# Attention with a matrix state and two MLP blocks on one core: queries transposed ahead of the kernel and loaded by DMA, in place of transposes on TensorE

## What is computed

```python
# q, k, v: (4, 8, 768, 48), beta: (4, 8, 768), all float32
k_n = k / (norm(k) + 1e-06)
for t in range(768):
    y[:, :, t] = q_t @ state                       # the queries read the state
    v_old = k_t @ state
    state = state + beta_t * outer(k_t, v_t - v_old)
# x = y, heads side by side: (4, 768, 384)
# block 1: mixing along the sequence (x^T U V), then relu(u @ w_ch1) @ w_ch2, both with residuals
# block 2: real part of a 2D FFT, layer norm, then the same kind of MLP
```

## Time and profile before

| | us |
|---|---|
| median of 3 runs | 1266.56 |
| lowest and highest run | 1260.3, 1274.25 |
| span of the profiled execution | 1268.3 |
| TensorE busy in it | 1173.2 |
| VectorE busy | 590.1 |
| ScalarE busy | 449.0 |
| GpSimd busy | 116.1 |

### The profile page before, as it was taken

The page is one execution under the profiler, slowest core; times in us unless marked ns, Lnnn a source line. Parts: engine busy times, 40 slices in busy tenths (PEclk is TensorE's granted clock), DMA queues, the critical chain, the costliest instruction groups (busy, mean ns, idle before and its releaser), DMA issues. The chain is left out here.

```text
span 1268.3 us, 24886 instructions
## 1 busy us (share of the span) xinstructions
PE 1173.2 (93%) x9978; PEld 1118.7 (88%) x9978; DVE 590.1 (47%) x1116; ACT 449.0 (35%) x853; POOL 116.1 (9%) x117
## 2 busy tenths in 40 slices
PE   4699999998999999599999999996799999999998
PEld 3598888888889888499999999995799999999998
DVE  7557776567764673352222222324553433434322
ACT  2566666565665653141211111212231221221211
POOL 4112211122111210000000000000000000000000
PEclk9899999999998997699999999998899999999999
DMA  5111112212112110441010100001111001001001
GB/s 98 26 32 34 31 26 37 39 26 39 22 33 39 51 62 29 127 151 52 1 38 1 37 0 0 1 1 52 48 52 38 19 1 38 19 0 37 19 16 40
DMA packets 98535, 44.87 MB, mean 35 GB/s; under 512 B 78037, under 2 KB 97162, under 8 KB 98314
## 3 DMA queue, kind: packets, MB, share of 16 engines
q1 hardware_dynamic: 98442, 43.47, 13.4%
HBM read 34.03 MB, written 11.85 MB: 36 GB/s over the span
## 5 line engine op out<-in xcount | busy, mean ns | idle before, releaser
L1220 DVE SCALAR_TENSOR_TENSOR hid_l_mix<-up_mix,hid_h_mix 128x384 fp32r<-128x384 f32 x96 | 53.4, 557 | 209.2 <-ACT hid_h_mix L1165 209.2
L382 DVE CAST_PREDICATED zi<-merge_mask,zb 128x512 f16<-128x512 uint8 x144 | 100.5, 699 | 98.8 <-PE zb L630 97.9
L1220 DVE SCALAR_TENSOR_TENSOR hid_l_dft<-up_dft,hid_h_dft 128x384 fp32r<-128x384 f32 x96 | 53.5, 557 | 183.9 <-ACT hid_h_dft L1165 183.8
L1165 ACT ACTIVATE hid_h_dft<-up_dft 128x384 fp32r<-128x384 f32 x96 | 47.2, 492 | 255.8 <-PE up_dft L1330 255.8
L1165 ACT ACTIVATE hid_h_mix<-up_mix 128x384 fp32r<-128x384 f32 x96 | 47.2, 492 | 245.7 <-PE up_mix L1330 245.7
L525 ACT CAST xi<-xb 128x512 f16<-128x512 f32 x144 | 82.3, 590 | 110.5 <-PE xb L656 68.8
L733 PE MATMUL pb<-kq_t,kz 128*128 128x256 f32 x384 | 99.2, 404 | 4.3 <-DVE nr L423 4.2
L1328 PE MATMUL dn_mix<-w2h_mix,hid_h_mix 128*128 128x384 f32 x288 | 99.5, 346 | 3.0 <-DVE hid_l_mix L1220 2.5
L1328 PE MATMUL dn_dft<-w2h_dft,hid_h_dft 128*128 128x384 f32 x288 | 98.5, 342 | 0.1
L1328 PE MATMUL up_mix<-act_h_mix,w1h_mix 128*128 128x384 f32 x288 | 97.1, 337 | 1.2 <-DVE act_l_mix L1238 1.2
L1328 PE MATMUL up_dft<-act_h_dft,w1h_dft 128*128 128x384 f32 x288 | 97.0, 337 | 1.2 <-DVE act_l_dft L1238 1.2
(11 more groups left out here) (170 smaller groups left out, 2476.8 us busy)
## 6 DMA issues: line engine op xcount, KB each, us to landing
k_raw<-k SPq DMA_DIRECT2D x24, 192.0 KB, 3.3
q_raw<-q SPq DMA_DIRECT2D x24, 192.0 KB, 3.5
v_in<-v SPq DMA_DIRECT2D x24, 192.0 KB, 3.2
stage_mix<-moe_w_ch SPq DMA_DIRECT2D x12, 384.0 KB, 4.5
stage_dft<-moe_w_ch SPq DMA_DIRECT2D x12, 384.0 KB, 3.8
x_rows<-x_sb SPq DMA_DIRECT2D x6, 384.0 KB
x_now_mix<-x_sb SPq DMA_DIRECT2D x4, 576.0 KB, 3.9
x_now_mix<-x_mem SPq DMA_DIRECT2D x4, 576.0 KB, 5.0
```

Of the source, the lines that this page charges most:

```text
L382: nc.vector.copy_predicated(blocks_all(zi[:, lv - 1, g], 1 << lv, 1), merge_mask[:, lv - 1].rearrange("p (n b) -> p n b", b=1 << lv), zb[g ...
L1165: nc.scalar.activation(hid_h[:, f % 2], up_b[f % 2][:, 0:HALF], ACT.Relu).then_inc(s_hh, 1)
L1220: nc.vector.scalar_tensor_tensor(hid_l[:, f % 2], up_b[f % 2][:, 0:HALF], 0.0, hid_h[:, f % 2], ALU.max, ALU.subtract).then_inc(s_hl, 1)
```

## The change

The queries are laid out anew in `kernel()`, by numpy on the host: from (4, 8, 768, 48) to (batch, chunk, o, d, p, position), where head = 2 p + o. One slice of it (one batch, one chunk, one o) is 48 rows of 4 x 128 numbers, 96 KB in one piece. Four DMAs a pair (two g, two o) write it into partitions 0 to 47 (o = 0) and 64 to 111 (o = 1) of `kq_t[:, 2 * par + g, :, 1]`, in runs of 128 numbers, 512 B. The tile `q_raw`, the query transposes on TensorE and the copies on ScalarE go. The partitions between are cleared once by VectorE, and SyncE waits for that once (`s_qpad`). The load of g waits for hop 5 of g two pairs before, since that reads the place it writes; it stands behind the load of `v_in` now. `gram(0, 0)` waits for all four loads of its pair.

```diff
-    q_raw = sb("q_raw", [C, 2, H, DP], F32)
...
-    s_q = sem("s_q")
+    s_q = [sem(f"s_q{n}") for n in range(2)]
+    s_qpad = sem("s_qpad")
...
-    PU = 14
+    PU = 12
...
             def load_rest(pair, par, c):
 
-                if needed(PU * (pair - 1) + 4):
-                    sp.wait_ge(s_pfull, PU * (pair - 1) + 4)
-                for g in range(2):
-                    sp.dma_start(q_raw[:, g, :, 0:D],
-                                 q[2 * par + g, :, bass.ds(c * C, C), :].rearrange("h p d -> p h d")).then_inc(s_q, 16)
-
                 if needed(2 * pair - 2):
                     sp.wait_ge(s_r, 2 * pair - 2)
                 for g in range(2):
                     sp.dma_start(v_in[:, 2 * par + g],
                                  v[2 * par + g, :, bass.ds(c * C, C), :].rearrange("h p d -> p h d")).then_inc(s_v[par], 16)
+
+                for g in range(2):
+                    if needed(12 * (pair - 2) + 8 + g + 1):
+                        sp.wait_ge(s_cfull, 12 * (pair - 2) + 8 + g + 1)
+                    for o in range(2):
+                        sp.dma_start(kq_t[DP * o:DP * o + D, 2 * par + g, :, 1],
+                                     q_t[2 * par + g, bass.ds(c, 1), o].rearrange("x d p t -> (x d) p t")).then_inc(s_q[par], 16)
...
+            sp.wait_ge(s_qpad, 1)
             load_rest(0, 0, 0)
...
-            for t in (k_raw, q_raw):
-                nc.gpsimd.memset(t[:, :, :, D:DP], 0.0).then_inc(s_pads, 1)
-            pool.wait_ge(s_pads, 2)
+            nc.gpsimd.memset(k_raw[:, :, :, D:DP], 0.0).then_inc(s_pads, 1)
+            pool.wait_ge(s_pads, 1)
...
+            nc.vector.memset(kq_t[:, :, :, 1], 0.0).then_inc(s_qpad, 1)
             nc.vector.memset(state[:], 0.0).then_inc(s_init, 1)
...
-                def queries(g):
-                    if not prep:
-                        return
-                    act.wait_ge(s_pfull, PU * pp + 2 + g + 1)
-                    nc.scalar.copy(kq_t[:, 2 * par + g, :, 1],
-                                   pb[g][:].rearrange("p (a t) -> p a t", t=C)).then_inc(s_pkq, 1)
-
...
-                def queries(g):
-
-                    if not prep:
-                        return
-                    pe.wait_ge(s_q, 32 * pp + 32)
-                    pe.wait_ge(s_pkq, 4 * pp + g + 1)
-                    turn_rows(pb[g], q_raw[:, g])
-
                 def gram(g, j):
                     if not prep:
                         return
                     for n in range(2):
 
                         if g == 0 and j == 0:
-                            pe.wait_ge(s_pkq, 4 * pp + 3 + n)
+                            if n == 0:
+                                pe.wait_ge(s_q[par], 64 * it + 128)
+                            pe.wait_ge(s_pkq, 2 * pp + 1 + n)
...
+    q = arrays.pop("q").reshape(B, HP, 2, NC, C, D)
+    arrays["q_t"] = np.ascontiguousarray(q.transpose(0, 3, 2, 5, 1, 4))
```

More of the change, by code:

```diff
@@ L105, in mirror_x, with attention @@
                  by_columns(x_rows[last:C * c + first - 1:-1, cols], 2)).then_inc(s_spill, 16)
-def attention(nc, ctx, x_sb, q, k, v, beta, cst, mem):
+def attention(nc, ctx, x_sb, q_t, k, v, beta, cst, mem):
     def sb(name, shape, dt):
@@ L419, in gram @@
                     for n in range(2):
-                        dve.wait_ge(s_pfull, PU * pp + 4 + 4 * g + 2 * j + n + 1)
+                        dve.wait_ge(s_pfull, PU * pp + 2 + 4 * g + 2 * j + n + 1)
                         for u in range(2):
@@ L542, in keys @@
                     if isinstance(s, int) and s == -2:
-                        act.wait_ge(s_pads, 5)
+                        act.wait_ge(s_pads, 4)
                     act.wait_ge(s_pfull, PU * pp + g + 1)
@@ L567, in n_turned @@
                         return
-                    act.wait_ge(s_pfull, PU * pp + 12 + g + 1)
+                    act.wait_ge(s_pfull, PU * pp + 10 + g + 1)
                     nc.scalar.copy(n_t[:, g], pb[g][:].bitcast(F16).rearrange("p (u n) -> p u n", n=C)).then_inc(s_pnt, 1)
@@ L588, in body @@
                 keys(1)
-                queries(0)
                 x_part(3, 0)
@@ L592, in body @@
                 x_part(3, 1)
-                queries(1)
                 x_part(4, 0)
@@ L612, in _ @@
             pe.wait_ge(s_beta, 2)
-            pe.wait_ge(s_pads, 5)
+            pe.wait_ge(s_pads, 4)
             def body(s, par, it):
@@ L1417, in mlp, with build @@
     pctx.close()
-def build(nc, q, k, v, beta, moe_U, moe_V, moe_w_ch1, moe_w_ch2, moe2_w_ch1, moe2_w_ch2,
+def build(nc, q_t, k, v, beta, moe_U, moe_V, moe_w_ch1, moe_w_ch2, moe2_w_ch1, moe2_w_ch2,
           c_gram, c_merge, c_first, c_ident, c_dft_s, c_dft_d, c_dft_r, out):
@@ L1432, in build @@
         with ExitStack() as own:
-            attention(nc, own, x_sb, q, k, v, beta,
+            attention(nc, own, x_sb, q_t, k, v, beta,
                       {"c_gram": c_gram, "c_merge": c_merge, "c_first": c_first, "c_ident": c_ident}, mem)
```

## The result

The changed kernel takes 1308.1 us (median of 4 runs, 1299.8 to 1313.3) against 1269.7 us of the kernel before on the same chips (median of 4, 1260.3 to 1274.3). The ratio is 1.030, with a 95% interval of 1.0245 to 1.0355. The prediction was 1280.4 us, range 1264 to 1298: the direction was right, the size was not; the loss is 38 us and not 14. The profiled execution spans 1306.1 us, before 1268.3, a difference of 37.8.

The account below looks back on a forecast made before the run. TensorE was taken to bound the kernel. Ten slots at 1.9 us of wait less 0.47 gained, +1.43 each, make +14.3; less 0.5 before the loop, +13.8 on 1266.6 gives 1280.4 us, range 1264 to 1298.

Parts of the forecast that it names:

- The order on TensorE: Behind hop 5 in slots 0 to 9, the Gram product, otherwise ready at T + 1.4, waits for all four loads.
- T: The end of `hop(5, 1)` on TensorE in a slot, from which the prediction counts the loads and the Gram product.
- The wait's length: At the Gram product: second load issued at T + 0.55, landing 2.7 us, start at T + 3.3, so 1.9 us idle.
- The gain: On TensorE in each slot, only the first four query transposes give time back: 0.47 us.
- exposed, and dearer: Rival, 0.20: clock falls in the new wait (+3 to +17 us on top) or landing nears the old load's; 1284 to 1302.
- Given back at the slot's end: Rival, 0.13: the 1.65 us wait for `state` at each slot's end shrinks; -3 us if all goes, +5 if half.
- Hidden after all: Rival, 0.10: landing by T + 1.4, or starting on g = 0's loads alone, leaves only gains, -6 us; 1252 to 1261.
- The slots before the loop: Slot -1 gains 0.5 us because a query copy ahead of ScalarE's `xi` copy goes; slot -2 gains nothing.
- SyncE's other work: Key loads and copies to memory move later at no cost; last copy some 19 us later, covered by more than 20.

Follow-up runs that it names:

- e2_split: The changed kernel with one semaphore for each pair parity and g, so each Gram product waits only for its own two loads: 1271.8 us, ratio 0.9996.
- e1_fill: The changed kernel with four matmuls, their result overwritten, just ahead of TensorE's wait for the queries in slots 0 to 9: 1282.9 us, 1.0132 times before.
- e6_waitonly: The kernel before, transposes kept, plus four unread query loads in runs of 2 KB and the wait for them: 1282.7 us, ratio 1.0108.
- e4_pad: The changed kernel with queries padded to 64 rows a half, one 256 KB load for each g in place of two of 96 KB: 1303.7 us, ratio 1.0261.
- e7_fill2: The changed kernel with two matmuls, their result overwritten, ahead of TensorE's wait for the queries: 1284.4 us, ratio 1.0112.

## Why the prediction was right and wrong

- **The order on TensorE** was right. The Gram product could start at T + 1.4, the new wait stands exactly there, ten times, and it is the wait for all four loads that exposes it: with the waits split it is gone (e2_split).
- **The wait's length** was 2.06 us and not 1.9, and the Gram product starts at T + 3.6 on average and not at T + 3.3. Errors in it partly cancel: the landing is 2.5 and not 2.7 us, but the second load is issued at T + 0.91 to T + 1.36 and not at T + 0.55. SyncE's first issue comes at T + 0.17 to T + 0.21 and not at T + 0.05, and the old load's pace of 0.5 us does not hold: here the second issue starts 0.74 to 1.16 us after the first.
- **The gain** was 0.37 us a slot by the distance of the v loads, forecast 0.47; why the other 0.1 is missing is not shown. The rule used, that the second transposes give back nothing because ScalarE's copy sets that point, held: `z_part(4, 1)` still waits 0.44 us for `xi`.
- **The step that failed** is the price put on the clock. The sum of +13.8 us has no term for it: the ten waits stand in it by their length alone. The fall was left to the rival "exposed, and dearer" and given 0.20 because 1.9 us are nearer to the 1.65 us wait that did no harm than to the 3.23 us wait behind which the clock fell. Two rows at either side do not tell where between them it turns; of the 40 waits of 1.7 to 2.4 us in four profiles it fell behind 30. The price of one fall was too low as well: 1.7 us was read from the one in the earlier trace rows, and four of the nine cost 3.4. The eight behind the waits of slots 1 to 8 cost 18.8 us and those at the loop's turns 3.4 more than before, together the 22.2 us; the rival's bound was 17 for ten. Its upper end of 1302 us is not the sum of its own terms either (1280.4 + 17 is 1297, and 1305 with the late landing); the measured 1308.1 lies above all of these. The forecast's own sum for what remains is close: e1_fill, with the clock held up, is 1.3% over before, where the sum was 1.1%.
- **Given back at the slot's end**: it did not happen; those waits are still 11.5 us. There are seven of them and not ten, so the rival was priced too high.
- **Hidden after all**: right in its condition (the loads of g = 0 alone are in time), not confirmed in its time: e2_split is at the time of before (0.9966 to 1.0026), not 6 us under it. Its profile has less clock than that of before; with the clock steadied in both kernels the gain is 3.9 us.
- **The slots before the loop**: -0.5 us was forecast. The v load of slot 0 came 1.8 us later in the first profile and at the same time in the second (76.67 and 74.94, before 74.92). There is no gain to be seen. In the first profile the clock stood at its lower level for 20.5 us ahead of that load, before for 13.7; whether that is the reason was not tested.
- **SyncE's other work** was covered, but by less than said: the last copy to memory was issued at 533.12, and the stage that reads it loaded at 549.35, 16 us later and not more than 20; the copy had moved by 50 us and not by the 19 and 14 forecast. GpSimd waits for the keys' load three times, 7.9 us in all, before three times and 7.3.

The Trainium skill (DMA: Bandwidth & Descriptors, Anatomy of one DMA) puts the fixed part of a transfer at about 2.0 us, most of it until completion is confirmed; its fit is for loads issued from GpSimd. An estimate by it is 2.2 us for 96 KB and 2.6 us for 256 KB. Measured on SyncE's queue are 2.1 us for 96 KB in runs of 2 KB (e6_waitonly), 2.5 in runs of 512 B, and 3.3 for 256 KB in runs of 512 B (e4_pad). The first agrees with the estimate; with runs of 512 B the landing is 0.3 and 0.7 us longer than that, and the measured figures stand. The Trainium skill (TensorE: Matmul & The Clock Gate, Part 1) also describes a clock that activity raises and idleness lowers; e1_fill agrees, since matmuls without use won 25 us. The last slot of before, busy for 20.00 of 20 us at 0.52, does not fit it as simply.

## What to carry to other kernels

Where TensorE sets the pace, price a new wait twice: by its length, and by the clock behind it. Here ten waits of 2 us cost 20 us themselves and some 22 us more through the clock, and a few matmuls that nobody reads took the second part away. Before moving work off TensorE onto a load, look for the last reader of the place that the load writes, and let each consumer wait only for the part it reads: one semaphore for all four loads was the difference between +38 us and 0.

## What the hardware showed that was not expected

- The granted clock falls behind pauses of about 2 us in an otherwise full stream: 30 of 40 waits of 1.7 to 2.4 us, 2 of 10 around 1.5, none of 20 with means of 1.1 and 1.3. In the two profiles of the changed kernel it fell behind different ones. The 1.65 us waits at the slots' ends never had it in the trace of before. What tells these from the 1.5 us waits is not settled.
- The clock can stand at its lower level while TensorE is busy without a pause: 493 to 513 in the trace of before (20.00 of 20 us busy, 0.52), when only the hops' products run, most of them with 64 columns to a matmul. In the changed kernel the same slot ran at full clock. Why it fell in the one and not in the other was not tested; it is worth about 8 us, the distance between 89.3 and some 81.5 us from the v load of slot 9 to the load of block 1 (before; e1_fill, e6_waitonly and e7_fill2).
- A DMA's issue on SyncE's queue and its landing both depend on the shape it writes: 96 KB to 48 partitions took 0.35 us to issue and landed after 2.1 us with one run of 2 KB a partition, 0.57 us and 2.5 us with four runs of 512 B (medians of e6_waitonly and of the changed kernel).
